# One table word per iteration chooses among six bodies in a block loop on ScalarE and VectorE

## What is computed

```python
def _moe2_ref(x, modality_id, w_gate, modality_bias, w1, w2):   # x: 3072 x 512, 8 experts, 1024 hidden
    logits = x @ w_gate + modality_bias[modality_id]
    e_idx = np.argmax(logits, axis=1)
    ...
    gate_w = probs[np.arange(N), e_idx]
    for e in range(E):
        mask = e_idx == e
        if not mask.any():
            continue
        h = np.maximum(x[mask] @ w1[e], 0.0)
        out[mask] = gate_w[mask, None] * (h @ w2[e])
```

## Time and profile before

| | |
|---|---|
| time, median of 3 runs | 1127.18 us (1126.96 to 1132.28) |
| the profiled execution, time | 1127.46 us |
| its span in the profile | 1125.9 us |
| TensorE busy, matmuls | 1017.9 us, 90% |
| VectorE busy | 729.1 us, 65% |
| ScalarE busy | 617.9 us, 55% |
| mean granted TensorE clock | 0.974 |
| raw weight pieces loaded | 16, of 512 KB: two turns |

### The profile page before, as it was taken

How to read it: one execution, slowest core, us unless ns; L and a number is a source line. 1 busy time by engine, 2 the same in 40 slices (tenths; PEclk the granted TensorE clock), 3 DMA queues, 4 the chain that set the end, 5 groups by cost and what they waited for, 6 DMA issues and landing times.

```text
span 1125.9 us, 24616 instructions
## 1 busy us (share of the span) xinstructions
PE 1017.9 (90%) x7840; PEld 667.3 (59%) x7840; DVE 729.1 (65%) x2393; ACT 617.9 (55%) x1425; POOL 399.3 (35%) x457
## 2 busy tenths in 40 slices
PE   1667888999999999999999999999899899789996
PEld 0544555565666566566566566655577677567774
DVE  6787977677977867887877786647673334533231
ACT  2676877665776666667667576536412233422221
POOL 3786876322335322425422232011132222132221
PEclk9967999999999999999999999999999999899999
DMA  9832111241212331221141120041015111101111
GB/s 289 281 90 64 34 34 34 62 123 34 63 34 58 68 94 34 59 71 34 35 93 37 34 63 1 1 167 40 20 39 189 48 47 47 33 29 53 41 54 38
DMA packets 24427, 75.14 MB, mean 67 GB/s; under 512 B 9680, under 2 KB 9808, under 8 KB 22800
## 3 DMA queue, kind: packets, MB, share of 16 engines
q1 hardware_dynamic: 15440, 60.58, 19.9%
q0 software_dynamic: 5728, 13.43, 3.7%
q10 hardware_dynamic: 3168, 0.02, 0.1%
HBM read 60.16 MB, written 14.12 MB: 66 GB/s over the span
## 4 chain that ended last, share of the span: by engine, by line
PE 63%; DVE 15%; issue 7%; ACT 7%; ACTq 3%; POOL 2%; DMA 1%; DVEq 1%; SPq 0%; POOLq 0%
PE h_ps L710 16%; PE acc L766 15%; PE pt_ps L1799 9%; PE h_ps L1851 5%; PE x_out L669 4%; PE acc L1851 3%; PE s_ps L546 2%; ACTq L1631 2%; PE pt_ps L615 2%; DVE qk_exp L398 2%; DVE g_raw L731 2%; DVE qk_top L389 1%; PE s_ps L815 1%; ACT probs L561 1%; DVE g_lo L751 1%
## 5 line engine op out<-in xcount | busy, mean ns | idle before, releaser
L766 PE MATMUL acc<-w_out_all,g_hi 128*128 128x512 f16 x768 | 228.3, 379 | 0.0
L710 PE MATMUL h_ps<-xt_hi,w_in_all 128*128 128x384 f16 x960 | 197.3, 329 | 13.2 <-DVE g_raw L731 13.2
L766 PE MATMUL acc<-w_out_all,g_lo 128*128 128x512 f16 x384 | 145.5, 379 | 5.2 <-DVE g_lo L751 3.6
L598 ACT ACTIVATE pt_hi<-pt_ps 128x256 f16<-128x256 f32 (+2 forms) x224 | 83.6, 380 | 109.4 <-PE pt_ps L615 104.8
L710 PEld LDWEIGHTS h_ps<-xt_hi,w_in_all 128*128 128x128 f16 x960 | 91.7, 98 | 67.6 <-issue 10.3
L99 POOL TENSOR_TENSOR tick<-tick 1x1 f32<-1x1 f32 x83 | 16.3, 196 | 291.0 <-ACT y L1867 132.1
L1816 DVE SCALAR_TENSOR_TENSOR hid_lo<-pt_ps,hid_hi 128x512 f16<-128x512 f32 x50 | 34.5, 691 | 130.3 <-ACT hid_hi L1813 124.9
L751 DVE SCALAR_TENSOR_TENSOR g_lo<-g_raw,batch_scale,g_hi 128x384 f16<-128x384 f32 x128 | 95.2, 744 | 33.1 <-ACT g_hi L741 30.7
L766 PEld LDWEIGHTS acc<-w_out_all,g_hi 128*128 128x128 f16 x768 | 75.0, 98 | 69.0
L602 DVE TENSOR_TENSOR pt_lo<-pt_ps,pt_hi 128x256 f16<-128x256 f32 (+2 forms) x224 | 94.3, 423 | 28.9 <-ACT pt_hi L598 27.4
L436 POOL TENSOR_TENSOR q_stack<-qk_raw,q_stack 64x768 f16<-64x768 f32 x31 | 50.8, 1640 | 165.5 <-ACT q_stack L432 165.5
(11 more groups left out here) (300 smaller groups left out, 2282.9 us busy)
## 6 DMA issues: line engine op xcount, KB each, us to landing
qk_raw<-in_qk SPq DMA_DIRECT2D x64, 454.0 KB, 6.0
raw<-in_w SPq DMA_DIRECT2D x16, 512.0 KB, 8.7
v_raw<-in_v SPq DMA_DIRECT2D x4, 1536.0 KB, 9.5
x_tokens<-x SPq DMA_DIRECT2D x24, 256.0 KB, 5.0
w_in_all<-in_w_in SPq DMA_DIRECT2D x4, 1024.0 KB, 12.9
w_out_all<-in_w_out SPq DMA_DIRECT2D x4, 1024.0 KB, 12.1
x_tokens<-g_raw SPq DMA_DIRECT2D x1, 1024.0 KB, 13.8
slots<-payload,dest POOLq DMA_INDIRECT x24
```

The source lines that it names most:

```text
L598: eng.activation(pt_hi[:, at, :], out, ACT.Copy).then_inc(q["pt_hi_done"], 1)
L710: mm = eng.matmul(h_of(m, f), w16[0][:, f, x * DM + k * P:x * DM + (k + 1) * P], r[:, par, k, :], start=(i == 0), stop=(i == 3 * KD - 1))
L766: mm = eng.matmul(acc[t][:, :], l[f % 2][:, t * P:(t + 1) * P], w16[1][:, f, x * DM:(x + 1) * DM], start=(f == 0 and i == 0), stop=(f == N ...
```

## The change

The plan gets a new row. `plan_late` writes, for each block, one word `event` from 0 to 5: 0 nothing, 1 look, 2 the next turn follows, 3 a turn has begun, 4 it began one iteration earlier, 5 look and 4 together. ScalarE and VectorE read this one word at the head of an iteration and run one of six bodies, each written out in full by `block_work` (for the even and for the odd iteration of a pass). The other words (the turn, the slot row, the turn to look at or to split) are read inside the bodies, where they are used; in a plain iteration that is one more word on each engine.

The look stands one iteration earlier where a turn has more than three blocks (in the last iteration but two), and its four pieces on each engine are set between the other steps instead of at the end. The slot load moves ahead of `transpose_x`. The experts of the turns, which only SyncE reads, get a table and a semaphore of their own, written by `plan_turns` behind the second `scale_x` of `joining_iteration`; `late_loads` waits for that.

```diff
     def plan_late(self, eng):
...
+        step(tt(sel[:, 0:w], now[:, 0:w], now[:, 3:w + 3], ALU.is_equal))
+        step(tt(sel[:, 0:w], sel[:, 0:w], first[:, 4:MB], ALU.mult))
+        step(tt(t[:, 0:w], first[:, 0:w], first[:, 3:w + 3], ALU.mult))
+        step(tt(sel[:, 0:w], sel[:, 0:w], t[:, 0:w], ALU.add))
...
+        step(ts(event, sel[:], 3.0, None, ALU.mult))
+        step(stt(event[:, 0:m], sel[:, 1:MB], 2.0, event[:, 0:m], ALU.mult, ALU.add))
+        step(stt(event[:, 1:MB], sel[:, 0:m], 4.0, event[:, 1:MB], ALU.mult, ALU.add))
+        step(tt(event[:, 1:MB], event[:, 1:MB], t[:, 0:m], ALU.add))
+        eng.tensor_copy(self.meta_late[:], metaf[:, 2:5, :]).then_inc(self.planned_late, 1)
+
+    def plan_turns(self, eng):
...
+    def block_work(E, eng, j, p, look=False, following=False, begun=False, earlier=False):
+
+        act, dve = E == "act", E == "dve"
+        if begun:
+            s = read(eng, 4, j, NE, lo=1)
+            eng.wait_ge(q["hid_mm"], 2 * j)
+            shared.split_w1(E, eng, s, 1)
+        if earlier:
+            t = read(eng, 4, j - 1, NE, lo=1)
+            eng.wait_ge(q["y_mm"], j - 1)
+            shared.split_w2(E, eng, t, 1)
+        relu(E, eng, j - 1, 1)
+        if dve:
+            output_part(E, eng, j - 1, 1 - p, turn_of(eng, j - 1))
+        if look:
+            n = read(eng, 2, j - 1, NE, lo=1)
+        if look and act:
+            shared.look_over(E, eng, n, 0)
+            shared.look_over(E, eng, n, 1)
+        if following:
+            s = read(eng, 4, j + 1, NE, lo=1)
+        scale_x(E, eng, j + 1, 1 - p)
+        if look and dve:
+            shared.look_over(E, eng, n, 0)
+        if following:
+            shared.set_scales(E, eng, s)
+        relu(E, eng, j, 0)
+        load_slots_again(E, eng, j - 1)
+        if look:
+            shared.look_over(E, eng, n, 2 if act else 1)
+        if following:
+            eng.wait_ge(q["hid_mm"], 2 * j + 1)
+            shared.split_w1(E, eng, s, 0)
+        if begun:
+            eng.wait_ge(q["y_half"], j)
+            shared.split_w2(E, eng, s, 0)
+        transpose_x(E, eng, j + 1, 1 - p)
+        output_scale(E, eng, j - 1, j - EARLY)
+        if look and act:
+            shared.look_over(E, eng, n, 3)
+        if look and dve:
+            shared.look_over(E, eng, n, 2)
+            shared.look_over(E, eng, n, 3)
+            shared.sum_rows(E, eng, n)
+        if act:
+            output(E, eng, j - 1, 1 - p)
+
     def iteration(E, eng, j, p, free):
...
-            begun, earlier = read(eng, 4, j, NE), read(eng, 4, j - 1, NE)
-            looking, following = read(eng, 2, j - 1, NE), read(eng, 4, j + 1, NE)
-            value = read(eng, 0, j - 1, NE * N - P) if E == "act" else turn_of(eng, j - 1)
-            next_turn_ends(E, eng, j, begun, earlier)
-            relu(E, eng, j - 1, 1)
...
-        if E == "act":
-            load_slots_again(E, eng, j - 1, value)
-            look_ahead(E, eng, looking)
-            output(E, eng, j - 1, 1 - p)
...
+            event = read(eng, 3, j, 5)
+            with eng.If(event < 1):
+                block_work(E, eng, j, p)
+            with eng.If(event > 0):
+                with eng.If(event < 2):
+                    block_work(E, eng, j, p, look=True)
+                with eng.If(event > 1):
+                    with eng.If(event < 3):
+                        block_work(E, eng, j, p, following=True)
+                    with eng.If(event > 2):
+                        with eng.If(event < 4):
+                            block_work(E, eng, j, p, begun=True)
+                        with eng.If(event > 3):
+                            with eng.If(event < 5):
+                                block_work(E, eng, j, p, earlier=True)
+                            with eng.If(event > 4):
+                                block_work(E, eng, j, p, look=True, earlier=True)
...
             scale_x(E, eng, j + 1, 1 - p)
+            shared.plan_turns(eng)
             relu(E, eng, j, 0)
...
-        eng.wait_ge(shared.planned_late, 1)
-        turns = read(eng, 3, NB, NE, lo=1)
+        eng.wait_ge(shared.planned_turns, 1)
+        turns = read_turns(eng, MB - 1, NE, lo=1)
```

More of the change, by code:

```diff
@@ L1356, in __init__ @@
         self.meta_late = sb("meta_late", [1, 3, MB], I32)
+        self.meta_turns = sb("meta_turns", [1, MB], I32)
         self.raw_in = [sem(f"raw_in{i}") for i in range(PIECES)]
@@ L1361, in __init__ @@
         self.planned_late = sem("planned_late")
+        self.planned_turns = sem("planned_turns")
+        self.turns_step = sem("plan_turns_step")
         self.late_step = sem("plan_late_step")
@@ L1392, in over_attention @@
         self.one_x = sb("one_x", [1, TURNS], F32)
[L1393 removed]
+        self.metaf = sb("metaf", [1, 6, MB], F32)
         self.per_turn = {n: sb("pt_" + n, [1, TURNS], F32) for n in "count blocks end active turn_end".split()}
@@ L1575, in plan_late @@
         step = chain(eng, self.late_step, 0)
-        tt, ts = eng.tensor_tensor, eng.tensor_scalar
-        mv, vec, grid, metaf = self.per_turn, self.vec, self.grid, self.metaf
[L1578 to L1586, removed]
@@ L1587, in plan_late @@
-        step(tt(metaf[:, 2, 0:w], vec["first"][:, 3:MB], b[:, 0:w], ALU.mult))
-        step(tt(metaf[:, 4, :], vec["first"][:], metaf[:, 1, :], ALU.mult))
-        step(tt(grid["a"][:], mv["turn_end"][:].unsqueeze(1).to_broadcast([1, MB, TURNS]), self.iota_j[:].unsqueeze(2).to_broadcast([1, MB, TURNS]), ALU.is_le))
+        tt, ts, stt = eng.tensor_tensor, eng.tensor_scalar, eng.scalar_tensor_tensor
+        mv, vec, metaf = self.per_turn, self.vec, self.metaf
+        first, now, b, t, sel = vec["first"], metaf[:, 1, :], vec["b"], vec["t"], vec["n"]
@@ new lines, in plan_late @@
+        look, event, begun = metaf[:, 2, :], metaf[:, 3, :], metaf[:, 4, :]
+        w, m = MB - 4, MB - 1
+        step(ts(b[:], now, 1.0, None, ALU.add))
+        step(ts(t[:], b[:], mv["turn_end"][:, TURNS - 1:TURNS], None, ALU.is_lt))
+        step(tt(b[:], b[:], t[:], ALU.mult))
+        step(tt(sel[:, 0:w], now[:, 0:w], now[:, 3:w + 3], ALU.is_equal))
+        step(tt(sel[:, 0:w], sel[:, 0:w], first[:, 4:MB], ALU.mult))
+        step(tt(t[:, 0:w], first[:, 0:w], first[:, 3:w + 3], ALU.mult))
@@ new lines, in plan_late @@
+        step(tt(sel[:, 0:w], sel[:, 0:w], t[:, 0:w], ALU.add))
+        step(ts(look, b[:], 0.0, None, ALU.mult))
+        step(tt(look[:, 0:w], sel[:, 0:w], b[:, 0:w], ALU.mult))
+        step(tt(begun, first[:], now, ALU.mult))
+        step(ts(sel[:], begun, 0.0, None, ALU.is_gt))
+        step(ts(t[:], look, 0.0, None, ALU.is_gt))
+        step(ts(event, sel[:], 3.0, None, ALU.mult))
+        step(stt(event[:, 0:m], sel[:, 1:MB], 2.0, event[:, 0:m], ALU.mult, ALU.add))
+        step(stt(event[:, 1:MB], sel[:, 0:m], 4.0, event[:, 1:MB], ALU.mult, ALU.add))
@@ new lines, in plan_late @@
+        step(tt(event[:, 1:MB], event[:, 1:MB], t[:, 0:m], ALU.add))
+        eng.tensor_copy(self.meta_late[:], metaf[:, 2:5, :]).then_inc(self.planned_late, 1)
+    def plan_turns(self, eng):
+        step = chain(eng, self.turns_step, 0)
+        mv, vec, grid, metaf = self.per_turn, self.vec, self.grid, self.metaf
+        over = [1, MB, TURNS]
+        step(eng.tensor_tensor(grid["a"][:], mv["turn_end"][:].unsqueeze(1).to_broadcast(over),
+                               self.iota_j[:].unsqueeze(2).to_broadcast(over), ALU.is_le))
@@ L1591, in plan_late @@
         step(eng.tensor_reduce(vec["n"][:], grid["a"][:], AX.X, ALU.add))
-        self.expert_of(eng, step, metaf[:, 3, :], vec["n"][:])
-        step(eng.tensor_copy(metaf[:, 3, NB:NB + 1], turns))
-        eng.tensor_copy(self.meta_late[:], metaf[:, 2:5, :]).then_inc(self.planned_late, 1)
+        self.expert_of(eng, step, metaf[:, 5, :], vec["n"][:])
+        step(eng.tensor_copy(metaf[:, 5, MB - 1:MB], mv["turn_end"][:, TURNS - 1:TURNS]))
+        eng.tensor_copy(self.meta_turns[:], metaf[:, 5, :]).then_inc(self.planned_turns, 1)
@@ L1626, in read, with read_turns @@
     def read(eng, row, j, hi, lo=0):
-        row_is_of_turns = row == 3
+        j = j - EARLY
         table, row = (shared.meta, row) if row < 2 else (shared.meta_late, row - 2)
-        j = j if row_is_of_turns else j - EARLY
         at = table[0:1, row, j:j + 1] if isinstance(j, int) else table[0:1, row, bass.ds(j, 1)]
+        return eng.value_load(at, min_val=lo, max_val=hi)
+    def read_turns(eng, at, hi, lo=0):
+        at = shared.meta_turns[0:1, at:at + 1] if isinstance(at, int) else shared.meta_turns[0:1, bass.ds(at, 1)]
         return eng.value_load(at, min_val=lo, max_val=hi)
@@ L1637, in load_turn @@
     def load_turn(eng, s):
-        e = read(eng, 3, s, NE - 1)
+        e = read_turns(eng, s, NE - 1)
         for i in range(PIECES):
@@ L1642, in load_turn @@
         shared.spread_by_dma(eng, dram, s)
[L1644 to L1674, removed]
     def early_rows(E, eng):
@@ L1817, in relu, with load_slots_again @@
```

(5 more changed lines are left out.)

9 lines of the change are left out of this document (removed).

## The result

The changed kernel takes 1176.61 us (median of 4 runs, 1174.55 to 1180.59) against 1128.37 for the kernel before in the same comparison: a ratio of 1.0426, 95% interval 1.0386 to 1.0466. It is slower by 4.3%, outside the predicted range and on the other side of no change. The mechanism is the prediction's first rival, fetches of code at every loop-back; its price was set far too low.

The account below looks back on a forecast made before the run. TensorE bounds the expert stage at 10.98 us per iteration, with 24.2 us of waits to win. Plain iterations -2.9, start -4.4, change of expert -6: -13.3 from 1127.46 gives 1114 us; range 1108 to 1140.

Parts of the forecast that it names:

- rival 1: Two code fetches of 1.8 us at each of ten loop-backs, +12 us: 1132.6 us, 1140 at 2.2 a fetch; chance 0.27.
- code loading: Fetching the longer loop's instructions: 1.8 us per fetch taken, from the small slot load's median 1.7; possibly hidden at loop-backs.
- 2.4 us to spare: ScalarE between y and ReLU at a loop-back: ReLU ready 1.55 us after y, 2.4 us before it is needed.
- which may stay in store: Argument against fetches at loop-backs: a plain iteration touches only three short places of code, which may remain held.
- Reads in plain iterations: Ahead of ScalarE's first ReLU: four table reads and one branch fewer; gain 2.9 us, bounds 0 to 2.9.
- The start: First two distances, 864 to 892: earlier slot load and four reads fewer; gain 4.4 us, between 3 and 5.4.
- The change of expert: Four distances, 947 to 1007: sum -7.1 us, taken as -6 for bodies entered first time; bounds -2.5 to -8.
- the 7.5 that the look was to give: First distance at the change of expert: four weight reductions moved to iteration 10, spread into gaps; gain 7.5 us.
- The new wait for `xg_lo`: Turn's last iteration: VectorE's new scales and low halves delay the next tokens, 12.6 against 10.98; new wait of 1.6 us.
- The 8.4 us of the prediction: VectorE's need in the turn's last iteration, from its ReLU through new scales, low halves and the tokens' low part.

Follow-up runs that it names:

- e3: Kernel before plus a never-entered block of 165 copies in VectorE's iteration (loop 227 to 561 instructions), ScalarE's loop unchanged: 1236.33 us, ratio 1.0962.
- e7: Kernel before plus a never-entered block of 100 copies in ScalarE's iteration (loop of 352 instructions): 1130.28 us, ratio 1.0021.
- e8: Kernel before plus a never-entered block of 115 copies in ScalarE's iteration (loop of 382 instructions): 1138.67 us, ratio 1.0103.
- e2: Kernel before plus a never-entered block of 130 copies in ScalarE's iteration (loop 149 to 412 instructions), VectorE's loop unchanged: 1174.80 us, ratio 1.0417.
- e4: Changed kernel with one body per iteration instead of six, rare parts under compares (loops of 203 and 289 instructions): 1116.12 us, ratio 0.9916 to before.
- e11: Changed kernel with one body, slot load put back behind the transposes and the tokens' split: 1118.74 us, ratio 0.9921 to before.
- e12: Changed kernel with one body, four more unused table words read at each iteration's head on both engines: 1132.98 us, ratio 1.0037 to before.
- e10: Changed kernel with one body, look put back in a turn's last iteration but one, pieces still spread: 1120.48 us, ratio 0.9931 to before.
- e1: Kernel before plus never-entered blocks in each iteration, 130 copies on ScalarE and 165 on VectorE (loops of 412 and 561): 1238.44 us, ratio 1.0981.

## Why the prediction was wrong

**The step that failed** is the one called code loading: no fetch at a loop-back is in the sum, and the 1.8 us per fetch of rival 1, with 2.4 us to spare, made them a loss of 12 us at a chance of 0.27. The place was right: two waits on ScalarE between y and the ReLU, once per loop-back, code packets inside the loop. The price was not. Alone a missed jump takes 2.2 to 3.3 us, one right behind another mostly 2.9 to 4.1 (2.43 and 3.65 on ScalarE, 2.33 and 3.62 on VectorE in e3), so the pair costs 6.1, not 3.6. Against 2.4 that is a stall of 3.2 to 3.7 rather than 1.2, and behind it came the lower clock (1.8 us more), which the rival mentions and does not add. The nearest row, a small load's 1.7 us, measured another thing: a jump that misses waits for more than one packet's transfer, which is about 0.6 us (an estimate: 0.5% of 16 engines' 1176 us, over 166 packets).

What I set against it, that a plain iteration touches only three short places "which may stay in store", is what e7, e8 and e2 refute: what counts is not how many instructions run but how long the loop is, with the parts that are jumped over, and the step from 1.0% to 4.2% takes thirty instructions. The absence of packets in the loop of before was read rightly, but it said only that 149 and 227 instructions fit, nothing of 413 and 561. The jumps missed on the way out of the loop (9.4 us) are in none of the cases. The range ended at 1140 although rival 1 reached 1150 by its own words; both are short of 1176.61.

The Trainium skill, "Runtime: NRT & Kernel Launch", section on instruction fetch mechanics, says that a taken branch outside of the held code waits for a DMA; the runs agree (2.82 us at e2's jump back). By its 512 instructions ScalarE's 413 could still have fitted; e8 and e2 put the border near 400 here. Its blocks of 16 KiB are what queue 8 brings (0.72 MB / 44), but queue 14, the one that grew, brings pieces of 8.2 KB, so for ScalarE and VectorE the measurement decides.

**The rest of the sum held in the main**, as e4 shows, which has the change without the long loop: 24.2 - 10.5 = 13.7 us gained in the 20 distances of its profiled execution against 13.3 forecast. By the medians the gain is 11.0, 1116.12 against the 1114 of the forecast. The terms one by one rest on a single execution each.

- Reads in plain iterations: 2.9 forecast, 2.9 gained; ReLU 1.42 us behind y, 1.55 forecast. In the changed kernel itself the distances without a loop-back show it (10.98 in the lines above).
- The start: 4.4 forecast, 5.4 gained. The reason was half wrong: I had counted on the earlier slot load as well, and e11 and e12 show that the reads do it without that. How much of the 5.4 is chance is open, with e7's 2.7.
- The change of expert: 6 forecast, 5.3 gained. The first distance falls from 18.5 to 11.0, the 7.5 that the look was to give; but in e10, with the look's pieces spread in its old iteration, it is 11.6, so the place of the look isn't what empties it. The new wait for `xg_lo` is there and longer than forecast, 3.1 us instead of 1.6. TensorE's timeline of e4 around it:

```profile
958.20 0.55 PE L1840 MATMUL h_ps<-ew_hi,hid_lo 128*128 128x512 f16 x1 [3.14 <-DVE xg_lo L1775]
...
973.76 0.39 PE L1840 MATMUL acc<-ew_hi,hid_lo 128*128 128x512 f16 x1 [2.75 <-DVE xg_lo L1775]
```

Here VectorE's splits hold the tokens back in two iterations in a row. VectorE's timeline ahead of the first of these waits, the new scales and the split:

```profile
950.82 0.42 DVE L1466 TENSOR_REDUCE both<-stats 128x2 f32<-128x256 f32 x1 [1.86 <-issue]
...
954.73 2.74 DVE L1486 SCALAR_TENSOR_TENSOR ew_lo<-raw,ew_scale,ew_hi 128x512 f16<-128x512 f32 x4 [1.34 <-ACT ew_hi L1482]
```

The 8.4 us of the prediction were read from the kernel before, where the split of the earlier trace rows found ScalarE's high halves ready. In e4 VectorE waits 1.34 us for them, and stands 1.86 for reads and compares where the sum had 1.3. The 1.34 and the 0.56 above the 1.3 make 1.9, near the 1.5 by which the wait is longer; no run took them away.

## What to carry to other kernels

Before writing a loop's body out several times, count the loop's instructions on each engine, alternatives included: the parts that are never entered count, and here the loss came at once when a border in the loop's length was passed. In a trace, look for packets on the code queue inside a steady loop and for a sequencer with 2 to 4 us of "issue" right around a loop instruction; the packets' share of DMA time was 0.5% here and said nothing. One body with the rare steps under a cheap test gave 0.8% here without the loss.

## What the runs showed of the hardware

- Code for ScalarE and VectorE arrived in packets of 8.2 KB (1.36 MB / 166) on queue 14, which alone grew in e2 (101 packets) and e3 (112). A loop of 382 instructions ran without fetching on ScalarE, a jump back over some 400 did not.
- A jump that missed stopped the sequencer for 2.2 to 3.3 us, and mostly 2.9 to 4.1 right behind another (after and e1 to e3; 5.2 and 5.1 once each in e1 and e3). Two engines that missed side by side cost little more than the worse one (51.9 us with both, 49.6 with ScalarE alone).
- A stall of TensorE of 3.2 us was followed by a granted clock of 0.64 over the next 3.1 us, which cost another 1.8. In e4 the wait of 3.14 was followed by 0.55 over 3.8 us, and that of 2.75 by full speed. Windows of e4 right behind each (columns as above; the second one begins 0.76 us ahead of the end of its wait):

```profile
958.20:962.00 3.80, 3.80 (x24) 2.67 (x25) 1.48 (x3) 2.92 (x5) 2.24 (x4) 0.55 0.17 66
973.00:977.00 4.00, 3.24 (x36) 2.44 (x37) 0.60 (x2) 1.81 (x3) 1.40 (x4) 1.00 0.02 4
```

Two waits of nearly one length, of which one cost more than itself: a stall is to be priced together with the granted clock read behind it.
